# Two kept columns for the first product of groups 4 and 5, and another order of the attention items

## What is computed

```
for t in range(768):
    cur = einsum(u * k[t], v[t])
    y[t] = einsum(r[t], state + cur)
    state = w[t] * state + einsum(k[t], v[t])
```

```
h = maximum(x @ w_in, 0)                      # 384 -> 1024
conv_out[s] = sum over k in 0..2 of conv_w[k] * h_padded[s + k]
x = (h * sigmoid(conv_out)) @ w_out           # 1024 -> 384
```

## Time and profile before

| | before |
|---|---|
| runs | 361.55, 357.62, 360.07 us; median 360.07 |
| profiled execution | 356.21 us, of which the span of instructions is 354.5 |
| busy PE | 333.5 us (94%) |
| busy DVE | 247.6 us (70%) |
| busy ACT | 145.1 us (41%) |
| busy POOL | 74.1 us (21%) |
| bytes moved by DMA | 22.79 MB, mean 64 GB/s |

### The profile page before, as it was taken

The page is one execution under the profiler, slowest core; times in us unless marked ns, Lnnn a source line. Parts: engine busy times, 40 slices in busy tenths (PEclk is TensorE's granted clock), DMA queues, the critical chain, the costliest instruction groups (busy, mean ns, idle before and its releaser), DMA issues.

```text
span 354.5 us, 8508 instructions
## 1 busy us (share of the span) xinstructions
PE 333.5 (94%) x3193; PEld 313.1 (88%) x3193; DVE 247.6 (70%) x523; ACT 145.1 (41%) x351; POOL 74.1 (21%) x138
## 2 busy tenths in 40 slices
PE   6877988999999799999899999899999999998996
PEld 6766867999999699999699999699999999997996
DVE  4997997977878767669779479767786612685212
ACT  2215984544266311266412157421265421663220
POOL 5633001144330222130205130204200030000300
PEclk9999998999999999999999999999999999999999
DMA  9998362822243610245305523501000010000101
GB/s 153 203 247 227 125 186 70 156 69 44 31 85 47 113 24 2 31 50 104 64 3 91 70 44 62 96 3 24 2 1 3 2 44 2 0 3 0 47 0 44
DMA packets 89251, 22.79 MB, mean 64 GB/s; under 512 B 83423, under 2 KB 87674, under 8 KB 89210
## 3 DMA queue, kind: packets, MB, share of 16 engines
q1 hardware_dynamic: 87984, 21.84, 30.6%
q10 hardware_dynamic: 1226, 0.41, 0.6%
HBM read 19.87 MB, written 2.36 MB: 63 GB/s over the span
## 4 chain that ended last, share of the span: by engine, by line
PE 80%; DVE 8%; issue 3%; SPq 3%; DMA 2%; POOL 2%; ACT 1%; DVEq 0%; POOLq 0%; ACTq 0%
PE hid L582 12%; PE hid L586 11%; PE hid L583 11%; PE acc L594 10%; PE acc L595 9%; PE acc L602 4%; PE acc L601 4%; PE pair_a L1320 2%; PE y_ps L1357 2%; DVE cg L1039 2%; SPq L695 2%; DVE stats L1219 2%; DVE cg L1223 1%; PE y_ps L1363 1%; PE y_ps L1369 1%
## 5 line engine op out<-in xcount | busy, mean ns | idle before, releaser
L1018 ACT ACTIVATE g_hi<-hid 128x256 fp32r<-128x256 f32 x64 | 24.6, 384 | 106.2 <-PE acc L602 94.1
L1250 DVE SCALAR_TENSOR_TENSOR g_lo<-hid,g_hi 128x256 fp32r<-128x256 f32 x64 | 26.8, 419 | 51.7 <-ACT g_hi L1018 51.5
L582 PE MATMUL hid<-xc_hi,w_hi 128*128 128x256 f32 x216 | 55.4, 288 | 2.5 <-ACT xc_hi L998 2.3
L583 PE MATMUL hid<-xc_hi,w_lo 128*128 128x256 f32 x216 | 53.0, 277 | 0.0
L1039 DVE SCALAR_TENSOR_TENSOR cg<-h_all,cols,cg 128x256 f32<-128x256 f32 x96 | 47.0, 490 | 6.2 <-ACT cg L967 5.5
L582 PEld LDWEIGHTS hid<-xc_hi,w_hi 128*128 128x128 f32 x216 | 40.6, 188 | 5.5 <-ACT xc_hi L998 3.7
L594 PE MATMUL acc<-w_hi,g_hi 128*128 128x384 f32 x128 | 43.9, 343 | 0.0
L595 PE MATMUL acc<-w_lo,g_hi 128*128 128x384 f32 x128 | 43.1, 337 | 0.0
L583 PEld LDWEIGHTS hid<-xc_hi,w_lo 128*128 128x128 f32 x216 | 40.6, 188 | 0.0
L582 PE MATMUL hid<-x_hi,win_hi 128*128 128x258 f32 x144 | 37.6, 289 | 1.0 <-ACT x_hi L928 1.0
L583 PE MATMUL hid<-x_hi,win_lo 128*128 128x258 f32 x144 | 36.8, 283 | 0.0
(11 more groups left out here) (188 smaller groups left out, 765.5 us busy)
## 6 DMA issues: line engine op xcount, KB each, us to landing
v_in<-in_v SPq DMA_DIRECT2D x12, 192.0 KB, 4.0
lent<-in_moe_w_ch SPq DMA_DIRECT2D x6, 384.0 KB, 3.2
out<-x SPq DMA_DIRECT2D x10, 192.0 KB, 1.9
lent<-in_moe_w_in SPq DMA_DIRECT2D x6, 256.0 KB, 4.5
lent<-in_moe_w_out SPq DMA_DIRECT2D x4, 384.0 KB, 5.8
w_two<-in_w SPq DMA_DIRECT2D x6, 192.0 KB, 4.9
k_two<-in_k SPq DMA_DIRECT2D x6, 192.0 KB, 5.1
ruk<-in_r SPq DMA_DIRECT2D x6, 192.0 KB, 2.9
```

The lines of the kernel that those rows point to most:

```text
L582: pe.matmul(out_ps, wh, xh, start=i == 0, stop=False)
L583: pe.matmul(out_ps, wl, xh, start=False, stop=False)
L1018: act.activation(relu_parts(n, j)[0], hid[j % 2][:, 0:GP], ACT.Relu)\
L1250: dve.scalar_tensor_tensor(out=low, in0=hid[j % 2][:, 0:GP], scalar=0.0, in1=high.bitcast(F32), op0=ALU.max, op1=ALU.subtract).then_inc(s_ ...
```

## The change

Two things change.

**First**, groups 4 and 5, the second and third group of the second sequence, no longer compute h for the two columns that the group in front of them has computed already. Their first product runs over the last 256 columns of the window (`begins(g)` is false for them) and the relu writes h from column 2 on. Columns 0 and 1 of h are columns 256 and 257 of the group in front: POOL copies those into a new tile `h_kept` [128, 8, 2] for groups 3 and 4 (`ends(g)` false), and back into the h buffer for groups 4 and 5. The copy back of a block waits for the same gate product as its relu and for the kept columns; the copy out waits for the relu. ACT's middle tap waits for the copy back (`s_back`), and a relu that takes over a buffer waits until its columns are kept (`s_kept`).

```diff
+        def begins(g):
+            return g < 4 or g * G % SEQ == 0
+        def ends(g):
+            return g < 3 or (g + 1) * G % SEQ == 0
...
+                elif kind == "hidden":
+                    j = item[2]
+                    q = n * JF + j
+                    h = h_sb[q % HBUFS]
+                    if not begins(n):
+                        pool.wait_ge(s_g, q - HBUFS + 1)
+                        pool.wait_ge(s_kept, kept(n - 1, j))
+                        pool.tensor_copy(h[:, 0:2], h_kept[:, j, :]).then_inc(s_back, 1)
+                    if not ends(n):
+                        pool.wait_ge(s_h, q + 1)
+                        if not begins(n):
+                            pool.wait_ge(s_back, returned(n, j))
+                        pool.tensor_copy(h_kept[:, j, :], h[:, GP:WIN]).then_inc(s_kept, 1)
...
+                    if q >= HBUFS and not ends((q - HBUFS) // JF):
+                        act.wait_ge(s_kept, kept((q - HBUFS) // JF, (q - HBUFS) % JF))
+                    if begins(n):
+                        act.activation(h_sb[q % HBUFS], hid[j % 2][:, 0:WIN], ACT.Relu).then_inc(s_h, 1)
+                    else:
+                        act.activation(h_sb[q % HBUFS][:, 2:WIN], hid[j % 2][:, 0:GP], ACT.Relu).then_inc(s_h, 1)
...
                     act.wait_ge(s_h, q + 1)
+                    if not begins(n):
+                        act.wait_ge(s_back, returned(n, j))
...
-                    last = hidden_passes(pe, hid[j % 2][:, 0:WIN],
+                    new = slice(0 if begins(n) else 2, WIN)
+                    last = hidden_passes(pe, hid[j % 2][:, 0:WIN - new.start],
...
-                                           x_hi[s][:, a, :], x_lo[s][:, a, :]) for a in range(KD)],
+                                           x_hi[s][:, a, new], x_lo[s][:, a, new]) for a in range(KD)],
```

**Second**, `FIRST` and `AFTER` hold the same 674 items in another order. Two lines of the table:

```diff
-            ("project2", 0, 4): [("weights", 19), ("mid", 4), ("r", 4), ("middle", 4), ("fetch", 21)],
+            ("project2", 0, 4): [("r", 4), ("middle", 3), ("fetch", 21), ("middle", 4), ("kv", 3)],
```

More of the change, by code:

```diff
@@ L379, in rwkv_mlp_kernel @@
             ("hidden", 1, 4): [("bv", 5)],
[L380 to L386 removed]
+            ("add", 0, 1): [("pads_r", 6), ("row_r", 6), ("middle", 6), ("row_k", 7)],
@@ L387, in rwkv_mlp_kernel @@
+            ("hidden", 1, 6): [("load_v", 6), ("k", 6)],
+            ("gate", 1, 5): [("ru", 6)],
+            ("conv", 1, 7): [("w", 6), ("ruk", 6)],
+            ("project", 1, 4): [("y", 5)],
             ("turn", 1): [("r", 6)],
-            ("hidden2", 1, 0): [("row_r", 7), ("scan1", 6)],
-            ("hidden2", 1, 2): [("scan2", 6), ("sums", 6)],
-            ("hidden2", 1, 3): [("bv", 6)],
-            ("project2", 1, 1): [("ru", 7)],
+            ("hidden2", 1, 0): [("scan1", 6), ("ru", 7)],
@@ new lines, in rwkv_mlp_kernel @@
+            ("hidden2", 1, 9): [("mid", 7)],
+            ("project2", 1, 7): [("sums", 7), ("mask", 7), ("ke", 6)],
+            ("hidden2", 1, 10): [("state", 6)],
+            ("project2", 1, 8): [("kv", 6), ("sc", 7)],
+            ("project2", 1, 10): [("bv", 7)],
+            ("hidden", 2, 1): [("load_w", 8)],
+            ("hidden", 2, 2): [("load_k", 8)],
+            ("project", 2, 0): [("middle", 7)],
+            ("conv", 2, 5): [("w", 8), ("load_r", 8)],
+            ("project", 2, 2): [("ke", 7)],
@@ L456, in rwkv_mlp_kernel @@
-            ("project", 4, 2): [("middle", 11)],
-            ("gate", 4, 5): [("bv", 11)],
-            ("hidden", 4, 7): [("y", 11)],
-            ("norm", 4): [("x", 11), ("late", 3, 9), ("late", 3, 10)],
+            ("turn", 2): [("kv", 7), ("k", 8)],
+            ("hidden2", 2, 0): [("ru", 9), ("r", 8)],
+            ("hidden2", 2, 1): [("row_r", 8), ("row_r", 9)],
+            ("project2", 2, 0): [("bv", 8), ("state", 7)],
+            ("hidden2", 2, 3): [("scan2", 8), ("mid", 8), ("middle", 8)],
@@ new lines, in rwkv_mlp_kernel @@
+            ("project2", 2, 8): [("bv", 9)],
+            ("hidden2", 2, 11): [("sums", 9)],
+            ("project2", 2, 9): [("mask", 9), ("kv", 8), ("sc", 9), ("load_w", 10), ("state", 8)],
+            ("project2", 2, 11): [("w", 10)],
+            ("conv", 3, 4): [("row_k", 10)],
+            ("gate", 3, 3): [("load_k", 10)],
+            ("project", 3, 1): [("ke", 9)],
+            ("hidden", 3, 5): [("middle", 9)],
+            ("conv", 3, 6): [("load_r", 10)],
+            ("hidden", 3, 7): [("row_r", 10)],
@@ new lines, in rwkv_mlp_kernel @@
+            ("conv", 3, 7): [("x", 9), ("y", 9), ("middle", 10)],
+            ("project", 3, 7): [("kv", 9)],
+            ("norm", 3): [("k", 10)],
+            ("turn", 3): [("ru", 10), ("scan1", 10), ("ruk", 10)],
+            ("hidden2", 3, 1): [("load_v", 10), ("state", 9)],
+            ("hidden2", 3, 2): [("scan2", 10), ("bv", 10)],
+            ("project2", 3, 0): [("sums", 10)],
+            ("hidden2", 3, 3): [("ru", 11), ("w", 11)],
+            ("project2", 3, 1): [("r", 10)],
+            ("hidden2", 3, 4): [("mid", 10)],
```

198 lines of the change are left out of this document (86 added, 112 removed).

## The result

The changed kernel takes 361.9 us as the median of 6 runs (361.7 to 362.6), where before has 359.03, a quotient of 1.008. The ratio on record, which goes by fast runs alone, is 1.0108, with a 95% interval of 1.0063 to 1.0154. Four more runs beside other kernels gave 362.1 and 1.0111 (1.004 to 1.018). The forecast was 357.8 us in a range up to 360.9, so both the sign and the range are wrong. The profiled execution has 361.7 us and a span of 360.0.

What follows compares the result with a forecast made beforehand. Bound by the DVE and POOL chain up to about 59 us, then by matmul count times spacing plus normalization gaps. Columns -1.04, order -0.35, start -0.9, copies 0 sum to -2.3: 360.07 to 357.8 us, range 355.1 to 360.9.

Steps and rivals of the forecast that it cites:

- order behind 60 us: Attention items on PE stand together more often, 27 interruptions of the other products instead of 32: -0.35 us.
- start: Before the first hidden at 32.02 us, a shorter DVE chain with fewer stretched scans: -0.9 us, bounds 0 and -1.5.
- I take -1.04, from the rows with the same count: First product of groups 4 and 5: 0.065 us a block saved, from comparison with nine second-product matmuls over 256 columns.
- rival A: First product of groups 4 and 5: two columns bring only their slope, -0.13 instead of -1.04; 358.7 us, chance 0.16.
- Rival C: Groups 4 and 5: GpSimd copies collide with DVE's two-operand instructions, making it slower; 361.6 us, chance 0.06.
- No new wait: Group 0's second half: kv 3 and state 3 come earlier, the relu residual on DVE ends as before; no cost.
- a wait of PE over 0.3 us inside 60 to 320: Outside the turns, such a wait would say the new order starves PE and the 0.35 us term is wrong.
- At worst +0.1: kv 7 moves from the gap before turn 2 to the one behind it: costed at 0, at most +0.1 us.
- price of an interruption: Attention items sc and ke on PE, apart against together: 1.71 against 1.64 us, so 0.07 us each.
- the first clash: DVE's scan at 13.85 us, stretched to 1.44 beside a POOL product; POOL idle under it would give -0.76 us.
- second clash: DVE's scan at 21.93 us, stretched by 0.83 beside a POOL product; gone if POOL is ahead, half taken, -0.4 us.
- Rival D: PE's clock, low in 52 to 56 us, may not fall there with the start shifted: -3.3 or more, 356.4 us, chance 0.13.

Runs made afterwards that it cites:

- columns_only: Kernel before with the 256 columns and the GpSimd copies alone, old order, h_kept allocated last; 358.08 us, ratio 1.0019.
- order_only: Changed kernel with 258 columns everywhere, no copies of kept columns, h_kept last, so the new order of items alone; 359.79 us, ratio 1.0029.
- first_only: Kernel before with the new list FIRST (the start) and its old table AFTER; 357.96 us, ratio 0.997, -1.04 us at equal clock.
- first_again: Second set of runs of the kernel before with the new list FIRST and the old table; 358.8 us, ratio 1.002, -0.92 us at equal clock.
- x_moved: Kernel before with one unused tile of 64 bytes a partition in front of xc_hi and xc_lo; 360.4 us, ratio 1.0058.
- kept_last: Changed kernel with h_kept allocated behind all other tiles, so xc_hi and xc_lo stand where they stood before; 359.66 us, ratio 1.003.
- order_mended: New order alone (258 columns everywhere) with pads_w 6 and kv 7 put back to their old places; -0.34 us at equal clock against before.
- all_moved: Kernel before with an unused 192-byte tile in front of win_hi, shifting everything from the weights on; one run, hidden2 at 113 ns a matmul, no time given.
- starts_b: Kernel before, old order, operands of hidden2 and the first product read from other starts by group; one run for spacing, no time given.
- w_moved: Kernel before with unused tiles putting all weights but the first product's at 64 modulo 256 bytes, xc unmoved; 360.93 us, ratio 1.0052.
- best: Changed kernel with the old table AFTER and tiles laid out so operands of groups 4 and 5 start at 64 modulo 256; 357.62 us, ratio 1.001.
- columns_placed: Kernel before with 256 columns and copies, groups 4 and 5 reading (other) columns from 64 modulo 256 bytes; 357.83 us, ratio 0.9974.
- pads_back: New order alone (258 columns everywhere) with pads_w 6 alone put back behind y 3; -0.40 us at equal clock against before.

## Why the prediction was wrong

Point by point, at equal clock:

| term | predicted | measured |
|---|---|---|
| narrower first product, with copies | -1.04 | +0.08 (columns_only; +0.39 against its own chip) |
| order behind 60 us | -0.35 | +1.0 (order_only less first_only and first_again) |
| start | -0.9 | -0.92 and -1.04 (first_again, first_only) |
| place of h_kept | not in the sum | +2.16 (x_moved) |
| share of low clock | not in the sum | +1.7 (not an effect at equal clock) |

The first four terms add to 2.2 us (2.8 with each against its own chip), against 1.7 and 1.9 measured; kept_last says that the fourth is nearer 1.5 in the changed kernel.

**The columns: the step "I take -1.04, from the rows with the same count" failed; it measured +0.08 us.** The prediction saw that 7 ns a matmul for two columns was far too much, named both explanations, and chose the wrong one; rival A was right. The row with the same count, a hidden2, differed in one more thing, the place of its operands against its weights, and that was all of it: over 256 columns at another place the trace of after has the spacing of 258. A like row with an unexplained 7 ns deserved no 0.49.

**The allocation was not costed at all.** The step that is missing would have stood under the copies. I read h_kept as 64 bytes of room; it moved xc_hi from 64 to 128 modulo 256, and 46 blocks lost the very 5 ns that the prediction meant to gain on 16. It had the number in hand: if hidden2 owes its 113 ns to where its rows start, then whatever moves them takes it away. Rival C, the slower one, had the right sign by a mechanism that did not happen: its 361.6 us is near the measured 361.9 by luck. By its own sum the copies of columns_only, 0.26 and 0.32 us in the mean, would have cost (0.58 - 0.33) x 8 = 2.0 us in group 4 alone.

**The order: the step "No new wait" failed; the table measured +1.0 us instead of -0.35.** I followed kv 3 and state 3 on DVE. I did not follow POOL, where a moved item that waits for PE (pads_w 6) stands ahead of middle 3. The sign that the prediction named, a wait of PE over 0.3 us inside 60 to 320, is there with 0.64 us in after. "At worst +0.1" for kv 7 is not decided by the runs: the turn ahead of it waits 1.1 us instead of 0.5 in after, but order_mended, with kv 7 back, gains no more than pads_back. The price of an interruption (0.07 us each, -0.35 in all) was tested by no run alone.

**The start was right in size, and in its mechanism for the first clash.** The scans and a product of the bonus on DVE and POOL, as in the earlier trace rows; of after:

```profile
13.43 0.67 DVE L1154 TENSOR_TENSOR_SCAN suf<-wz,open 128x261 f32<-128x261 f32 x1
...
17.48 0.55 DVE L1188 TENSOR_REDUCE bonus<-ruk 128x8 f32<-128x384 f32 x1 [0.23 <-POOL ruk L779]
...
21.03 0.74 DVE L1151 TENSOR_TENSOR_SCAN pre<-wz,open 128x260 f32<-128x260 f32 x1
```

```profile
14.69 1.00 POOL L765 TENSOR_TENSOR ruk<-r_two,u_all 128x384 f32<-128x384 f32 x1 [1.73 <-DVE bonus L1188]
```

```profile
30.83 0.36 PE L599 MATMUL hid<-x_hi,win_hi 128*128 128x258 f32 x1 [0.97 <-ACT x_hi L959]
```

The scan of tile 1 is down from 1.44 to 0.67 us, ru 1 starts at 14.7 (predicted 14.5), sums 1 runs at 17.5 (17.4), and the first hidden starts at 30.83 (31.1), against the earlier trace rows. k 1 was not late. The scan of tile 1 is short in all nine traces with the new start and stretched (1.43 or 1.44) in all eight with the old one. The second clash is gone too (0.74), but that half of the term is less sure than it looks: it is missing in four of the eight traces with the old start as well (x_moved, columns_only, all_moved, starts_b). Nor does one start of hidden carry a size: it lies at 31.2 to 34.2 us in the traces with the old start and at 30.8 to 32.7 with the new one, with medians of 32.1 and 31.1. The size is that of first_only and first_again, which do not separate the clashes from the other moves of the start.

**The copies were right at 0, within a few tenths.** They are 0.24 and 0.27 us each, and no project of groups 4 and 5 waits in after.

**The clock was named on one side only.** Rival D let it fall less (its -3.3 would be 356.8 us, not the 356.4 given); it fell more often, behind the normalizations of groups 1 and 2. The 3.9 us between the profiled execution and the median, carried over as a constant, fit such a difference of clock: that execution had 0.995 and none of these drops, and later runs of before near 360.1 us mostly list 0.981. The ten runs of the changed kernel have a mean of 0.9805, kept_last, the same program with xc moved back, 0.9848, and x_moved, before with xc moved away, 0.9871. No single part brings the 0.9805, the same drops stand in traces of both orders (columns_only, kept_last, w_moved, best), and ten runs are few where before spreads from 0.972 to 1.000. So whether the change lowers the clock at all, and by what, stays open, and with it half of the loss.

## What to carry over

A new tile is not free where TensorE reads what stands behind it: if two equal matmuls of a kernel differ in spacing by a few ns, note where their moving rows start against their weights, and keep it through every edit of the allocation, or allocate new tiles last. When a table moves an item, follow what stands behind it on every engine on which it waits, the small copies on GpSimd first. And where runs spread with the granted clock, compare at equal clock: here that cut the scatter of repeated runs from 2.0 us to 0.5; compare with the runs of the same chip, which differed by up to 0.4 us.

## What the runs showed of the hardware

- Matmuls in float32r over 256 columns can follow each other at 113 ns when the moving row starts 64 bytes short of the weights modulo 256; at all ten other starts tried it is 117 to 120 ns. Over 258 columns it is 119 to 122 ns from any start seen, and over 384 columns mostly 173 to 178. The Trainium skill, TensorE: Matmul & The Clock Gate, section Back-to-back issue gap, gives N/2.4 + 2.5 ns as the gap of an isolated matmul, 109 ns for 256 columns as an estimate from the page. For a stream of weight loads and matmuls, as here, it gives about 131 ns at 512 columns. The rows here follow neither: 113 ns at best for 256 columns, and 173 already for 384. Why this distance is the fast one is not shown, nor why group 5 needed four blocks to reach it in columns_placed and best.
- A drop of the clock in a normalization gap lasts beyond it: in after hidden2 0 to 2 of group 1 run at 213 ns a matmul in the median, against 118 behind them. Over all runs, 0.01 less of mean clock goes with 2.57 us more.
- A DVE scaling with one tensor input and a scalar for each partition, 0.42 us in before and first_only, took 1.04 us beside a GpSimd product in pads_back and 0.55 to 0.88 in five other traces with the new table, where it overlaps that product less. So not only the scans with two inputs are held up.
